# Last pair's tails first, three tiles routed beside its last units, and the slot loop's boundary behind the second layer's products

## The reference

```python
scores = q @ k.T / sqrt(64)
scores = where(scores >= max(scores) - tau, scores, -1e9)
attn = exp(scores - max(scores)); attn /= sum(attn) + 1e-9
x = (attn @ v), heads side by side: [2304, 512]

logits = normalised(x) @ normalised(expert_emb).T / moe_tau     # 8 experts
e = argmax(logits); gate = softmax(logits)[e]                   # top 1
x = gate * (relu(x @ w1[e]) @ w2[e])

h = x @ w_in
out = (max(h, 0) + alpha * min(h, 0)) @ w_out
```

## Time and profile before

| | us |
|---|---|
| median of three runs | 1055.79 (1053.36 to 1055.9) |
| profiled execution | 1049.71 |
| its span | 1048.0 |
| PE busy in it | 1018.3 (97%) |
| DVE, ACT, POOL busy | 528.6, 391.0, 336.3 |
| mean granted clock of PE | 0.991 |

### The profile page before, as it was taken

How to read it: one execution, slowest core, us unless ns; L and a number is a source line. 1 busy time by engine, 2 the same in 40 slices (tenths; PEclk the granted TensorE clock), 3 DMA queues, 4 the chain that set the end, 5 groups by cost and what they waited for, 6 DMA issues and landing times.

```text
span 1048.0 us, 19527 instructions
## 1 busy us (share of the span) xinstructions
PE 1018.3 (97%) x6559; PEld 893.6 (85%) x6560; DVE 528.6 (50%) x1203; ACT 391.0 (37%) x814; POOL 336.3 (32%) x443
## 2 busy tenths in 40 slices
PE   8899999999999699999999999999999999999997
PEld 7788898898898578888888878999999899999996
DVE  5778887987987312222221326644444444444442
ACT  5677676776776032222222323221111121111211
POOL 2233334312113596799776361010010010100101
PEclk9999999999999799999999999999999999999999
DMA  5765767767562655465535245000000000000000
GB/s 157 174 140 121 196 168 190 173 161 216 122 143 87 218 191 187 136 199 196 204 127 198 99 164 169 31 25 9 29 31 31 1 30 30 30 0 0 31 1 30
DMA packets 103502, 116.36 MB, mean 111 GB/s; under 512 B 70268, under 2 KB 70300, under 8 KB 102916
## 3 DMA queue, kind: packets, MB, share of 16 engines
q1 hardware_dynamic: 88228, 87.51, 30.2%
q10 hardware_dynamic: 11056, 13.69, 4.1%
q0 software_dynamic: 4144, 14.20, 3.8%
HBM read 68.53 MB, written 18.82 MB: 83 GB/s over the span
## 4 chain that ended last, share of the span: by engine, by line
PE 85%; DMA 4%; DVE 4%; SPq 4%; issue 1%; ACT 1%; POOL 0%; ACTq 0%; POOLq 0%; DVEq 0%
PE bank L682 75%; PE bank L685 9%; DMA k_st<-k_both 3%; SPq L435 1%; SPq L446 1%; DVE probs L1301 1%; DVE neg_max L1293 1%; DVE q_lo L1318 0%; DMA y_sorted<-x_sorted 0%; DMA x_sorted<-X,pos 0%; ACT q_hi L1083 0%; DMA x_row<-x_sorted 0%; SPq L414 0%; SPq L453 0%; SPq L474 0%
## 5 line engine op out<-in xcount | busy, mean ns | idle before, releaser
L682 PE MATMUL bank<-x_hi,ring 128*128 128x384 f32 x768 | 210.8, 337 | 1.3 <-DVE act L1648 1.3
L682 PE MATMUL bank<-ring,g_hi 128*128 128x512 f32 x576 | 179.1, 392 | 0.0
L1235 ACT ACTIVATE g_hi<-act 128x384 fp32r<-128x384 f32 x96 | 50.4, 525 | 303.3 <-DVE act L1648 300.9
L585 POOL TENSOR_TENSOR ring<-stage,ring 128x2048 fp32r<-128x2048 f32 x32 | 147.1, 4598 | 4.8
L682 PEld LDWEIGHTS bank<-x_hi,ring 128*128 128x128 f32 x768 | 140.3, 188 | 5.0 <-DVE act L1648 1.6
L1645 DVE TENSOR_SCALAR neg<-bank,alpha_col 128x384 f32<-128x384 f32 x96 | 59.2, 617 | 144.0 <-PE bank L682 144.0
L682 PE MATMUL bank<-x_lo,ring 128*128 128x384 f32 x384 | 128.9, 336 | 0.0
L1293 DVE TENSOR_REDUCE neg_max<-bank 128x1 f32<-128x576 f32 x144 | 104.3, 753 | 38.0 <-PE bank L682 37.0
L682 PEld LDWEIGHTS bank<-ring,g_hi 128*128 128x128 f32 x576 | 106.8, 188 | 18.7 <-DVE g_lo L1596 0.3
L1067 ACT ACTIVATE probs<-bank,neg_max 128x576 f32<-128x576 f32 x144 | 103.1, 740 | 48.9 <-DVE neg_max L1293 48.8
L682 PE MATMUL bank<-k_st,q_st 128*128 128x288 f32 (+5 forms) x696 | 114.7, 306 | 3.7 <-DVE probs L1301 3.4
(11 more groups left out here) (183 smaller groups left out, 1416.7 us busy)
## 6 DMA issues: line engine op xcount, KB each, us to landing
stage<-in_moe_w SPq DMA_DIRECT2D x32, 1024.0 KB, 5.5
k_st<-k_both SPq DMA_DIRECT2D x60, 288.0 KB
x_row<-x_sorted ACTq DMA_DIRECT2D x23, 296.0 KB, 2.9
y_sorted<-y_row ACTq DMA_DIRECT2D x21, 256.5 KB, 2.6
q_st<-q_hi SPq DMA_DIRECT2D x30, 160.0 KB
q_st<-q_lo SPq DMA_DIRECT2D x30, 160.0 KB
qraw<-in_q SPq DMA_DIRECT2D x16, 256.0 KB, 3.2
vraw<-in_v SPq DMA_DIRECT2D x16, 256.0 KB, 4.9
```

The lines of the kernel that those rows point to most:

```text
L585: nc.gpsimd.tensor_tensor(lo, src, hi.bitcast(F32), ALU.subtract).then_inc(piece_lo, 2)
L682: return nc.tensor.matmul(dst, lhsT, rhs, start=start, stop=stop)
L1235: nc.scalar.activation(g_hi[f % 3][:, :], act2[f % 2][:, :], ACT.Copy).then_inc(g_hi_ready, 1)
```

## The change

What it does, part by part:

- In the last pair the units are taken in the order tail, 0, 1, 2, 3 (`unit_at`); numbers of tiles and transposes follow (`short`, `last_main`).
- The tail rows lie in tiles 12 and 13. Group 3 has three tiles (13, 14, 15) and wants units 0 to 2 of the last pair's order and all tail stores; group 4 has two (16, 17). On DVE group 3's steps stand before the last two `normalise`, on PE `rank(3)` before the last `turn_out`. SP issues both tail stores of the last pair.
- `WARM` is 34 instead of 26, and seven more such products stand behind slot 0's transposes.
- On PE a pass of the slot loop now begins with the transposes and last two chunks that belong to the slot before (`slot_last(i-1)`), and ends with `second_first` (`slot_first(i)`); the last slot's number and expert are read behind slot 1. `EARLY` is 15 instead of 16.
- `copy_y` and `store_y` of the last slot move into group 0 of the last stage, and the split of w_out begins with one piece before it on ACT and none on DVE.

```diff
-EARLY = MIN_SLOTS - 2
+EARLY = MIN_SLOTS - 3
...
-WARM = 26
+WARM, WARM_SPLIT = 34, 7
...
-ROUTES = ((0, 4), (4, 4), (8, 5), (13, 4), (17, 1))
-TAIL_TILES = (12, 17)
+ROUTES = ((0, 4), (4, 4), (8, 5), (13, 3), (16, 2))
+TAIL_TILES = (12, 13)
...
-        r_keep = {nt: at(f"r_keep{nt}", [P, EXPERTS * (nt + 1)]) for nt in (1, 4, 5)}
+        r_keep = {nt: at(f"r_keep{nt}", [P, EXPERTS * (nt + 1)]) for nt in (2, 3, 4, 5)}
...
+        def unit_at(n, j):
+
+            return (j + UNITS - 1) % UNITS if n == PAIRS - 1 else j
+
+        def is_tail(n, j):
+            return unit_at(n, j) == MAIN
...
+        def last_main(n, j):
+
+            m, i = before(n, j)
+            return last_main(m, i) if is_tail(m, i) else (m, i)
...
-        def for_slots(eng, body):
+        def for_slots(eng, body, between=None):
...
             body(1, True)
+            if between:
+                between()
             with eng.Fori(2, EARLY) as i:
...
-            sp.wait_ge(x_ready, UNITS * PAIRS)
-            store_tail(sp, PAIRS - 1, (0,))
+            sp.wait_ge(x_ready, UNITS * (PAIRS - 1) + 1)
+            store_tail(sp, PAIRS - 1, (0, 1))
...
             turn_out(last_pair, UNITS - 2)
+            rank(3)
             turn_out(last_pair, UNITS - 1)
-            rank(3)
             rank(4)
...
+            def half_of(i):
+                return expert_of(i)[1]
+
+            def slot_first(i):
+
                 e, half_at = expert_of(i)
                 if not static(i):
                     e_before, half_before = expert_of(i - 1)
                 if static(i):
                     turn_slot(0)
+                    warm_up(WARM_SPLIT)
                 pe.wait_ge(piece_lo, e * PIECES + DC)
                 pe.wait_ge(xs_lo, i + 1)
                 first(half_at, 0)
                 first(half_at, 1)
                 if not static(i):
                     second_first(i - 1, e_before, half_before)
+
+            def slot_last(i, half_before, more=True):
+
                 if more:
                     turn_slot(i + 1)
                 turn_h(i, 0)
...
+            def slot(i, more):
+
+                if not static(i):
+                    slot_last(i - 1, None if static(i, 1) else half_of(i - 2))
+                slot_first(i)
...
-            last_slot = pe.value_load(slot_count[0:1, 1:2], min_val=MIN_SLOTS - 1, max_val=SLOTS - 1)
-            e_last, half_last = expert_of(last_slot)
-            for_slots(pe, slot)
+            late = []
+
+            def load_last():
+                i = pe.value_load(slot_count[0:1, 1:2], min_val=MIN_SLOTS - 1, max_val=SLOTS - 1)
+                late.extend((i, *expert_of(i), half_of(pe.snap(i - 1))))
+
+            for_slots(pe, slot, load_last)
+            last_slot, e_last, half_last, half_before_last = late
+            slot_last(last_slot, half_before_last)
...
-            act.wait_ge(x_ready, UNITS * PAIRS)
-            store_tail(act, PAIRS - 1, (1,))
...
-                    if static(g) and f < PIECES - 2:
-                        late_hi_parts(2 + f, 3 + f)
+                    if static(g) and f < PIECES - 1:
+                        late_hi_parts(f + 1, f + 2)
+                    if static(g) and f == 1:
+                        store_y(last_slot)
...
-            late_hi_parts(0, 2)
-            store_y(last_slot)
+            late_hi_parts(0, 1)
...
             normalise(PAIRS - 1, UNITS - 3)
-            normalise(PAIRS - 1, UNITS - 2)
-            normalise(PAIRS - 1, UNITS - 1)
             for k in range(7):
                 route_step(3, k)
+            normalise(PAIRS - 1, UNITS - 2)
             route_step(3, 10)
             for k in (7, 8, 9):
                 route_step(3, k)
+            normalise(PAIRS - 1, UNITS - 1)
             for k in range(10):
                 route_step(4, k)
...
-            copy_y(last_slot, LAST_BANK)
...
+                    if static(g) and f == 0:
+                        late_lo_parts(0, 1)
                     low(g, f)
-                    if static(g) and f < PIECES - 2:
-                        late_lo_parts(2 + f, 3 + f)
+                    if static(g) and f == 0:
+                        copy_y(last_slot, LAST_BANK)
+                    if static(g) and 0 < f < PIECES:
+                        late_lo_parts(f, f + 1)
...
-            late_lo_parts(0, 2)
+            dve.wait_ge(late_hi, 1)
             group(0, 0, True)
```

More of the change, by code:

```diff
@@ L303, in build, with heads_of, short @@
         o_stored = [sem(f"o_stored{i}") for i in range(GT)]
+        def unit_at(n, j):
+            return (j + UNITS - 1) % UNITS if n == PAIRS - 1 else j
+        def is_tail(n, j):
+            return unit_at(n, j) == MAIN
+        def heads_of(n, j):
+            return (0,) if is_tail(n, j) else (0, 1)
+        def short(n, j):
+            return 1 if n == PAIRS - 1 and j else 0
         def tile_no(n, j, h=0):
-            return TILES_PAIR * n + 2 * j + h
+            return TILES_PAIR * n + 2 * j + h - short(n, j)
         def turn_no(n, j, w):
-            return TURNS_PAIR * n + (3 * j + w if j < MAIN else 3 * MAIN + (1 if w else 0))
+            return TURNS_PAIR * n + 3 * j - short(n, j) + (w if not is_tail(n, j) else 1 if w else 0)
+        def last_main(n, j):
+            m, i = before(n, j)
+            return last_main(m, i) if is_tail(m, i) else (m, i)
         def before(n, j):
@@ L353, in rest @@
                 with eng.If(end > i + 1):
-                    body(i, i + 1 < SLOTS)
+                    body(i, True)
                     if i + 1 < SLOTS:
@@ L606, in small_steps @@
                 for j in range(UNITS):
-                    for h in heads_of(j):
+                    for h in heads_of(n, j):
                         pool.wait_ge(max_ready, tile_no(n, j, h) + 1)
@@ L728, in scores @@
                 if not (static(n) and j == 0):
-                    last_no = tile_no(n, j - 1, h) if j else (tile_no(n - 1, MAIN) if h == 0 else tile_no(n - 1, MAIN - 1, 1))
+                    last_no = tile_no(*last_main(n, j), 1) if h else tile_no(*before(n, j))
                     pe.wait_ge(probs_ready, last_no + 1)
@@ L736, in scores @@
                     jobs = []
-                    for x in (heads_of(0) if j == MAIN else (h,)):
+                    for x in ((0, 1) if u == MAIN else (h,)):
                         for part in range(2):
@@ L784, in values @@
                 tail = probsT[buf][:, 2 * MAIN * P:2 * SEQ]
-                if j < MAIN:
+                if not is_tail(n, j):
                     for c in range(CHUNKS):
@@ L843, in pair @@
                         scores(*nxt, 0)
-                    if more and nxt[3] < MAIN:
+                    if more and not is_tail(nxt[0], nxt[3]):
                         scores(*nxt, 1)
@@ L886, in _, with warm_up @@
             turn_out(last_pair, UNITS - 2)
+            rank(3)
             turn_out(last_pair, UNITS - 1)
-            rank(3)
             rank(4)
             pe.wait_ge(piece_lo, PIECES)
-            for _ in range(WARM):
-                mm(bank[:, M_BANK, :], ring[:, 0, 0:P], ring[:, 0, 0:D], True, True)
+            def warm_up(n):
+                for _ in range(n):
+                    mm(bank[:, M_BANK, :], ring[:, 0, 0:P], ring[:, 0, 0:D], True, True)
+            warm_up(WARM)
             H_BANK, HT_BANK, X_BANK, Y_BANK = (0, 1), (2, 3), 4, 5
@@ L1328, in normalise @@
                 got = bank[:, turn_bank(n, j), TURN_AT:TURN_AT + TURNED]
-                if j < MAIN:
-                    at_x = x_tile(n, j) * XC + n % 4 * TURNED
+                if not is_tail(n, j):
+                    at_x = x_tile(n, unit_at(n, j)) * XC + n % 4 * TURNED
                     V.tensor_tensor(X[:, at_x:at_x + TURNED].rearrange("p (h d) -> p h d", h=2),
```

34 lines of the change are left out of this document (15 added, 19 removed).

## The result

The changed kernel takes 1045.1 us (median of four, 1043.9 to 1046.2) against 1054.6 for the kernel before on the same occasion: ratio 0.991, 95% interval 0.9889 to 0.9931, so 7 to 12 us faster. I had forecast 1050.4, faster by 5.4, with a range that ended at 1047.2. The direction was right, the size was not: 1.8 times as much came. (The forecast counts from a median of 1055.79; 1.2 us of its 5.3 us distance to 1045.1 are that median alone, which was 1054.6 here.) The two profiled executions, though, differ by 5.0 (spans 1048.0 and 1043.0), close to the forecast. That gap between the profiles and the medians is what had to be explained.

The account below looks back on a forecast made before the run. PE, busy 97% of the 1048.0 us span, was taken as the bound, leaving only its idle and half-clock time. -2.7 (slots to last stage) and -2.7 (attention to slot 0) took 1055.79 to 1050.4; range 1047.2 to 1054.8.

Parts of the forecast that it names:

- The exit: Slots to last stage: PE's jump out of nested Ifs, about 2.8 us, 1.42 idle; 18 products hide it: -1.42.
- The other idle: Last stage: PE's 1.27 us wait for act before hidden 2 goes once the last y's copy moves: -1.27.
- The offset from span to median: Whole kernel: the median, 1055.79, lies 6.1 us above the profiled execution; this difference was carried over to the forecast.
- Attention to slot 0: Stretch from the end of attention to the start of the slots: -2.7 us, bounds -1.2 to -3.6.
- The +0.2 for two tails in a row: End of attention: pair 15's tail follows pair 14's, PE stalls 0.65 us, the last unit's scores start 0.2 later.
- Last scatter: POOL before slot 0: the last of five scatters begins at 350.7 us instead of 353.58: -2.9.
- The tail store: Last unit of attention: DVE may stand 0.6 to 1.3 us for it, mostly covered; if nothing covers it, +1.3.
- The warm products: PE before slot 0: 34 take 10.6 us if cold, 7.9 if warm; slot 0's products then run at full clock.
- the cold case of my bounds: Before slot 0: PE at half clock, warm-up ends at 359.5, transposes gain only 1.5 us, slot 1 comes 2.2 sooner.
- One half fails: Rival, 24%: the start gives only 1.2 us, or the exit idle stays (-1.3, not -2.7); total -3.9 to -4.0, 1051.8.
- both fail: Rival, 13%: both stretches fall short, or run to run spread hides the gain: -2.5 us in all, 1053.3.
- Slower: Rival, 7%: the slot loop's boundary loses its cover in 20 slots; at 0.5 us a slot +4.6, 1060.4.

Follow-up runs that it names:

- short: Kernel before with the bound on the number of slots set to 22 instead of 25: 1056.6 us against 1056.62, ratio 0.9999.
- again: Kernel before, without an edit, timed and profiled once more: 1056.29 us against 1055.84, ratio 1.0003.
- tail: Kernel before with only the last pair's order and the routing changed, 26 warm products kept: 1054.2 us against 1055.84, ratio 0.9976.
- shortlasty: Kernel before with the bound of 22 slots and the last y's copy and store moved into the last stage: 1050.7 us against 1056.62, ratio 0.9956.
- slot: Kernel before with only the slot loop's boundary moved on PE (EARLY 15): 1053.8 us against 1055.84, ratio 0.9986.

## Why the prediction was wrong in size

**The exit: this step failed.** I wrote "The exit is covered by six products (1.40 us) and costs 1.42 beyond them, so about 2.8 us". The mechanism was right: the idle is the jump out of the nested Ifs and not the second hT_lo, as `short` shows, and a boundary behind 18 products hides all of it. Its price was read from one execution, which was a cheap one. In four of seven profiles it is about 3.7 us idle and then half clock for the next products, which adds 1.55 us in again and 2.4 in tail. That an idle time could halve the clock behind it I had weighed for slot 0 and not here. The whole stretch, from the last slot's first hT_lo to hidden 2, was 13.7 us in the first profile. In the six profiles with old exit and old y copy its mean is 16.1, and after the change it is 10.86: 1.0 to the end of the last six products, then 5.7 for 24 products of the last slot and 4.2 for 24 hidden ones. That is **-5.3** where I had -2.7. The other idle, 1.27 before act, is the same stretch: it shrinks to 0.55 where the exit is dear, since the y store has then landed before PE's last product and the copy waits for PE.

**The offset from span to median: the same fault once more.** I carried over all of the 6.1 us between the first profile's execution and the median. It was no constant. That execution lay at the fast end of before: of the 35, 15 and 23 runs timed later the fastest are 1051.1, 1051.6 and 1049.9. Part of its lead was in attention (pair 14's tail at 332.06, in the other profiles at 332.7 to 338.1; the nine with the old order have 333.9 on the mean, so 1.9), of which the change removes nothing; 0.6 was in the stretch to slot 1 (41.02 against 41.62), and 2.4 was the cheap exit (13.7 against 16.1), which the change removes. A stated spread of 2.5 us in the runs was a hint that some stall differs from run to run. I had taken it for noise around my sum.

**Attention to slot 0: the mechanism right, the size short.** Forecast -2.7. The first pair of profiles has 41.02 - 37.73 = 3.3 behind the common event; against the mean of nine old ones (41.62) it is 3.9. The +0.2 for two tails in a row lies ahead of that event. It can be read from the distance between the tails of pair 13 and pair 14: 18.37 to 18.40 us in the nine profiles with the old order, 18.67 to 18.69 in the five with the new one, so +0.3; PE's stall there is 0.44 in the changed kernel, where I had 0.65. The stretch gained 3.0 by the first pair of profiles and 3.6 by the mean. By steps:
- Last scatter: forecast -2.9, measured 21.52 - 18.73 = -2.8.
- Positions: forecast 349.3, that is 17.0 after pair 14's tail (332.06 and the +0.2); measured 350.44, 17.1.
- The tail store: I let DVE stand up to 1.3. It didn't stand at all; its x_tail_sb begins at 337.08, right behind the maxima.
- The warm products: ran at half clock until about 354.8, took 10.24 (forecast 10.6), and held the transposes back: the transposes came 2.2 us sooner and not 2.9 (28.97 to 26.77 after pair 14's tail). This was the cold case of my bounds.
- Slot 1: I had -2.2 for the cold case, the +0.2 included; on that count the first pair of profiles has -3.0. Of the difference 0.5 is that the transposes came sooner than that case had them (26.8 after pair 14's tail, forecast 27.2), 0.3 that slot 1's rows came 8.0 us after them and not 8.27, and 0.2 that PE began 2.97 after the rows and not 3.14, less 0.1 for the two tails in a row.

**The rivals.** "One half fails" and "both fail" didn't happen: the exit idle went. "Slower", a stall at each pass of the loop, didn't happen either: 250.8 us in all profiles. The page rule that I weighed (the Trainium skill, "Runtime: NRT & Kernel Launch", "Instruction fetch mechanics") says that a taken branch to code outside the pages held has to fetch it first. `short`, where no idle time is left once nothing is jumped over, agrees. The traces also show fetches of instructions. In the four dear exits two packets of 16 KB start within 0.13 us of each other around the last slot's first hT_lo and take 1.65 to 2.03 us each. In the three cheap ones they start 3.1 to 3.2 us apart and take 0.9 to 1.7; the five profiles with the moved boundary have them 4.9 to 5.2 apart, and short and shortlasty have only one of them there.

**Sum.** -3.9 + 0.3 - 5.3 = -8.9, from profiles alone; the medians say -9.5 and -8.3. Against the first profile alone, whose exit was cheap, the same steps are -3.3 + 0.3 - 2.85 = -5.85, near the -5.4 forecast: the working fits the execution that it was read from. That the two profiled spans differ by only 5.0 comes from attention, 1.0 us later in the second one for a reason that is not the change.

**Luck.** That all of the dear exit is hidden was not in my sum. Six products (1.4 us) and 3.7 of idle time are an estimated 5.1, and I had put only 4.2 us of products in front of the branch, so a dear exit should still show 0.9. None of the five profiles with the moved boundary shows any idle time. Either the dear form doesn't arise there, which the distance of the two fetches would fit, or the estimate is too high; no run separates the two.

**Open.** Why the exit is dear in one execution and cheap in the next: the load of w_out begins at the same distance from it in both kinds. That two fetches at the same time hinder each other goes with the dear exits in all seven profiles, but no run sets it, and each fetch is only about 1 us longer where the idle time is 2.2 longer. Why attention differs by up to 5 us at pair 14 was not followed either. And the seven products behind slot 0's transposes were not tried apart from the eight more before them.

## What to carry to other kernels

Before a stall of one profile is given a price, profile the unchanged kernel three or four times: a stall with two sizes looks like a constant in one profile. Where the profiled execution lies well below the median, the difference is stalls too, and a change may remove them. An idle time that is moved and not removed can cost more at its new place: in short it halved the clock there. Two waits in one stretch, of which each takes up what the other gives free, can't be judged apart: each part alone gave about 2 us, both together 5.5, though the intervals don't rule out plain addition.

## What the runs showed of the hardware that I had not expected

- A jump out of nested Ifs over three bodies of a slot costs PE by estimate either about 2.8 or about 5.1 us: 1.37 to 1.65 or 3.56 to 3.77 of idle time behind 1.4 us of products; jumps of the loop itself, every 12.5 us, show nothing.
- An idle time of 3.56 to 3.77 us has half clock behind it in every one of five profiles (the four dear exits, and short before hidden 2); one of 1.37 to 1.65 us in none of three, and none follows one of 2.73 (slot). Two that stand close together, 1.30 and 1.75 us with 0.66 us of transposes between them, have it behind them too (before slot 0, first profile: 0.50 granted over 364 to 366 us).
- A store of a few KB (y_sorted<-x_sorted) landed 4.9 and 5.3 us after its issue (first profile, slot), and 5.85 in short, while a load of 1 MB was under way; the one before it, issued before that load, had landed in 2.35 and 2.4 us (first profile, slot).
